# Features 128 to 191 of the output stacked by token halves before they are transposed, in a fused two-layer float32 kernel on one Trainium2 core

## The reference

```python
w = softmax(weight)                        # [8, 7], one row per 24 features
x = causal_conv7(x, w).reshape(8192, 192)
h = x @ w_in1;  x = (h / (1 + exp(-1.702 * h))) @ w_out1     # 192 -> 2048 -> 192
h = x @ w_in2
P = a[0] + a[1]*h + a[2]*h**2 + a[3]*h**3
Q = 1 + abs(b[0])*abs(h) + abs(b[1])*h**2
return (P / (Q + 1e-6)) @ w_out2           # [8192, 192]
```

## Time and profile before

| | |
|---|---|
| median of 3 runs | 1399.64 us (1399.02 to 1403.59) |
| profiled execution | 1398.76 us, span of its instructions 1396.6 us |
| granted TensorE clock, mean | 0.997 |
| PE, PEld, DVE, ACT, POOL busy | 1328.7, 706.6, 1107.6, 972.0, 326.5 us |

### The profile page before, as it was taken

The page is one execution under the profiler, slowest core; times in us unless marked ns, Lnnn a source line. Parts: engine busy times, 40 slices in busy tenths (PEclk is TensorE's granted clock), DMA queues, the critical chain, the costliest instruction groups (busy, mean ns, idle before and its releaser), DMA issues. The chain is left out here.

```text
span 1396.6 us, 14941 instructions
## 1 busy us (share of the span) xinstructions
PE 1328.7 (95%) x4896; PEld 706.6 (51%) x4896; DVE 1107.6 (79%) x1205; ACT 972.0 (70%) x1113; POOL 326.5 (23%) x150
## 2 busy tenths in 40 slices
PE   2999999999999999999999999999999999999886
PEld 1455555554555555555554555555455555555332
DVE  5229788887888888888888888888888888877885
ACT  4337777677777777677777767777677777766774
POOL 4202222222222222222222222222222222222222
PEclk9999999999999999999999999999999999999998
DMA  8100000000000000000000000000000000000000
GB/s 209 36 12 0 12 1 23 1 23 1 12 11 0 23 0 20 3 11 11 0 23 0 12 10 3 20 0 23 0 12 12 0 12 1 12 0 12 0 12 11
DMA packets 32884, 20.37 MB, mean 15 GB/s; under 512 B 10322, under 2 KB 30802, under 8 KB 32850
## 3 DMA queue, kind: packets, MB, share of 16 engines
q1 hardware_dynamic: 32372, 19.93, 5.2%
q10 hardware_dynamic: 477, 0.01, 0.0%
HBM read 13.64 MB, written 6.29 MB: 14 GB/s over the span
## 5 line engine op out<-in xcount | busy, mean ns | idle before, releaser
L675 POOL TENSOR_TENSOR work<-work 128x1024 f32<-128x1024 f32 x128 | 303.7, 2373 | 1013.2 <-ACT work L432 1010.1
L271 PE MATMUL acc_a<-g,down 128*128 128x512 f32 x1024 | 477.4, 607 | 0.0
L271 PEld LDWEIGHTS acc_a<-g,down 128*128 128x128 f32 x1024 | 183.4, 190 | 292.5 <-issue 292.5
L570 DVE TENSOR_TENSOR work<-work,h 128x1024 f32<-128x1024 f32 x128 | 156.3, 1221 | 195.8 <-ACT work L432 195.7
L277 PE MATMUL acc_b<-g,down 128*64 128x512 f32 x1024 | 270.9, 606 | 30.0 <-DVE x_a_lo L588 16.0
L428 ACT ACTIVATE work<-h,par 128x1024 f32<-128x1024 f32 x128 | 142.6, 1114 | 195.8 <-PE h L265 195.8
L257 PE MATMUL h<-x_a_hi,up_a_hi 128*128 128x512 f32 x512 | 234.6, 458 | 25.4 <-DVE x_b L560 16.8
L456 ACT ACTIVATE work<-work 128x1024 f32<-128x1024 f32 x128 | 135.9, 1061 | 156.1 <-POOL work L675 154.1
L258 PE MATMUL h<-x_a_lo,up_a_hi 128*128 128x512 f32 x512 | 201.2, 393 | 0.0
L259 PE MATMUL h<-x_a_hi,up_a_lo 128*128 128x512 f32 x512 | 200.6, 392 | 0.0
L260 PE MATMUL h<-x_b,up_b_hi 128*128 128x512 f32 x512 | 200.4, 392 | 0.0
(11 more groups left out here) (74 smaller groups left out, 967.4 us busy)
## 6 DMA issues: line engine op xcount, KB each, us to landing
out<-y_out SPq DMA_DIRECT2D x16, 384.0 KB, 2.5
x_in_a<-in_x SPq DMA_DIRECT2D x16, 256.0 KB, 2.8
down<-in_moe_w_out SPq DMA_DIRECT2D x8, 384.0 KB, 6.3
x_in_b<-in_x SPq DMA_DIRECT2D x32, 64.0 KB, 2.6
work<-in_moe_w_in SPq DMA_DIRECT2D x8, 256.0 KB, 6.0
work<-in_moe_w_in SPq DMA_DIRECT2D x16, 128.0 KB, 6.3
wts<-in_weight ACTq DMA_DIRECT2D x2, 0.4 KB
wts<-in_weight SPq DMA_DIRECT2D x2, 1.3 KB
```

The costliest lines, as they stand in the source:

```text
L271: last = mm(l.acc_a[:], l.down[:, f, 0:P], l.g[:, slot, k, :], start=f == 0, stop=f == STEPS - 1)
L570: tt(tu, tu, h, ALU.mult).then_inc(t2_ready, 1)
L675: tt(m, sq[(s - LAG_RATIO) % 2], seed, ALU.mult).then_inc(m_ready, 1)
```

## The change

`y_b` becomes 128 rows by 256 columns: rows 0 to 63 hold features 128 to 191 of tokens 0 to 255 of the tile, rows 64 to 127 the same features of tokens 256 to 511. Two copies of 64x256 on ACT fill it, and acc2_read counts to three a tile. Half h of a tile is then blocks 2h and 2h+1 for y_a, and columns 128h to 128h+127 of y_b, which hold blocks h and h+2: `transpose_y` has three transpositions of 128 columns and no product. ACT empties `turned` with two copies, 128x256 for the a part of blocks 2h and 2h+1, and 128x128 for the b part of blocks h and h+2, and y_ready counts to four a tile. The memset and its semaphore go.

```diff
-        y_b = sb("y_b", [P, NT])
+        y_b = sb("y_b", [P, HALF])
...
-                    wait(sp, y_ready, 2 * (i - 1))
+                    wait(sp, y_ready, 4 * (i - 1))
...
             def transpose_y(tile, half):
 
-                if isinstance(tile, int) and tile == 0:
-                    pe.wait_ge(y_b_cleared, 1)
-                wait(pe, acc2_read, 2 * (tile + 1))
+                wait(pe, acc2_read, 3 * (tile + 1))
                 for j in range(2):
-                    toks = slice((2 * half + j) * P, (2 * half + j + 1) * P)
-                    nc.tensor.transpose(turned[:, j * D:j * D + P], y_a[:, toks], ident[:])
-                    last = mm(turned[:, j * D + P:(j + 1) * D], y_b[:, toks], ident[:, 0:DB], start=True, stop=True)
-                last.then_inc(y_transposed, 1)
+                    block = 2 * half + j
+                    nc.tensor.transpose(turned[:, j * P:(j + 1) * P], y_a[:, block * P:(block + 1) * P], ident[:])
+                nc.tensor.transpose(turned[:, 2 * P:3 * P], y_b[:, half * P:(half + 1) * P], ident[:])\
+                    .then_inc(y_transposed, 1)
...
-                        wait(pe, y_ready, 2 * (tile - 3))
+                        wait(pe, y_ready, 4 * (tile - 3))
...
-                    wait(pe, y_ready, 2 * (i - 2) + half)
+                    wait(pe, y_ready, 4 * (i - 2) + 2 * half)
...
-                        wait(pe, acc2_read, 2 * (i - 1))
+                        wait(pe, acc2_read, 3 * (i - 1))
...
-                    fn(y_out[:, 2 * half:2 * half + 2, :],
-                       turned[:, 0:2 * D].rearrange("p (j d) -> p j d", d=D), ACT.Copy).then_inc(y_ready, 1)
+                    fn(y_out[:, 2 * half:2 * half + 2, 0:P],
+                       turned[:, 0:2 * P].rearrange("p (j d) -> p j d", d=P), ACT.Copy).then_inc(y_ready, 1)
+                    fn(y_out[:, half::2, P:D],
+                       turned[:, 2 * P:3 * P].rearrange("p (j d) -> p j d", d=DB), ACT.Copy).then_inc(y_ready, 1)
...
-                    fn(y_b[0:DB, :], acc_b[0:DB, :], ACT.Copy).then_inc(acc2_read, 1)
+                    fn(y_b[0:DB, :], acc_b[0:DB, 0:HALF], ACT.Copy).then_inc(acc2_read, 1)
+                    fn(y_b[DB:P, :], acc_b[0:DB, HALF:NT], ACT.Copy).then_inc(acc2_read, 1)
                     fn(y_a[:], L2.acc_a[:], ACT.Copy).then_inc(acc2_read, 1)
...
-            nc.vector.memset(y_b[DB:P, :], 0.0).then_inc(y_b_cleared, 1)
```

More of the change, by code:

```diff
@@ L163, in build_program @@
         s2_ready = sem("s2_ready"); z1_ready = sem("z1_ready"); z2_ready = sem("z2_ready")
-        g2_ready = sem("g2_ready"); g2_used = sem("g2_used"); y_b_cleared = sem("y_b_cleared")
+        g2_ready = sem("g2_ready"); g2_used = sem("g2_used")
         acc2_read = sem("acc2_read"); y_transposed = sem("y_transposed"); y_ready = sem("y_ready")
```

## The result

The changed kernel takes 1392.92 us (median of 6 runs, 1391.17 to 1396.26) against 1400.25 us before (6 runs): a ratio of 0.9948, 95% interval 0.9933 to 0.9963, or 7.3 us less. The forecast was 9.0 us less, 1390.6 us. The change makes the kernel faster, by the mechanism that was named, and by four fifths of the size.

A forecast was written before the change was run, and what follows sets the result against it. PE's own list bounds the kernel until about 1290 us. 28 halves x 0.33 gain 9.2 us, the tail loses 0.2; 1398.76 minus 9.0 is 1389.8, plus 0.9 to the median: 1390.6 us, range 1387.8 to 1394.4.

The forecast's parts named there:

- What bounds the kernel: Up to about 1290 us the time is the length of PE's own list; whatever leaves the list leaves the time.
- the rival of the hidden gain: A chain of ACT, POOL and DVE sets the period, so the gain is hidden: 1399.8 us, chance 0.02.
- Step 1: PE, y's transposition: two products (0.43 us) become one transposition (0.105); 0.33 us a half, 28 halves, 9.2 us gained.
- The rival that its price would be a product's: On PE, y_b's transposition costs what a float32 product costs: 6.2 us gained, 1393.6 us, chance 0.05.
- Step 2: ACT, y_b in two copies of 64x256: 0.40 us each, 0.80 instead of 0.48, 0.32 us more.
- Step 3: PE's first L277 of the next step waits for y_a: slack 0.30 us against 0.32 added, 0.02 x 14, nothing.
- Step 4: ACT, y_out in two copies per half: 0.1 us more overlapped, 0.4 without overlap; hidden from PE.
- Step 5: DVE loses one memset at the very start, needed only some 190 us later: nothing.
- Step 6: The end, ACT on the path: tile 14's copies +0.32, tile 15 together -0.14; tail +0.2 us.

The follow-up runs named there:

- the run with the split wait: Changed kernel, down projection's wait split: y_b's copies before the first L277, y_a only before layer 2's first L271; 1393.67 us, ratio 0.9948; repeated: 1391.01 us.
- the padded run: Kernel before, each product of y_b replaced by a transposition of all 128 rows (64 to 127 zeros), y_b not stacked; 1392.16 us, ratio 0.9953.
- the run with ACT's part alone: Kernel before, PE's list unchanged, y_b in two copies of 64x256 on partitions 0 to 63, y_out in two per half; 1398.9 us, ratio 0.9998.
- second profile: Changed kernel run once more, unedited; 1392.21 us, ratio 0.9956, span 1389.7 us.
- The stacked product: Changed kernel with the third transposition replaced by a float32 product of the stacked y_b with the whole identity; 1394.28 us, ratio 0.996.

## Why the prediction was right, and where its sizes were off

- **What bounds the kernel: right.** PE's list did. Every profiled span moved by what the run changed in the periods, within 0.9 us, and the rival of the hidden gain falls: steps of 10.47 went to 10.17 and stayed there.
- **Step 1, 0.33 us a half: measured 0.30** (28 halves give 8.4 us in the run with the split wait, where nothing else disturbs them; 9.2 were forecast). The price of the removed products (0.43 us) holds, since the padded run's 0.64 to 0.41 follows from it. The third transposition was forecast at 0.105 us and takes 0.12 to 0.13: 28 x 0.03 = 0.8 us less than forecast, the largest single miss of the sum. The rival that its price would be a product's fails; a product there costs 0.22.
- **Step 2, 0.32 us more on ACT for y_b: measured 0.31.** The reading that neighbours don't overlap where the starting partition changes was drawn from L441 and L411, and the run with ACT's part alone shows the contrast (0.26 against 0.39). The Trainium skill's bubble (Advanced Engine Details and Errata, The Read-Write Bubble) is visible here only at such a change. The Trainium skill (ScalarE: Activation LUTs, Rules for kernel authors) budgets about 0.3 us per ACTIVATE and 0.83 ns per element; for 256 columns that is 0.51 us, an estimate, against 0.36 to 0.38 measured; the 0.54 us that the two pages together gave is too much.
- **Step 3, the slack of 0.30 us: the size that failed relatively most.** Forecast 0.02 us x 14 = nothing; measured, the step is 0.03 to 0.04 us longer in ten tiles and 0.13 to 0.15 in four, 0.8 to 0.9 us together, of which some 0.4 us is left after the following steps. y_a's own copy became 0.02 us longer (0.60 after a copy to other partitions); that makes the usual tile's loss. The slack was read from one tile, and the four are other tiles: 0, 11, 12 and 13, whose copies stand outside the hardware loop. There L277 followed y_a's end by only 0.30 us in the kernel before, not by the 0.35 of tile 7, the one that was read:

```profile
1090.44 0.58 ACT L469 ACTIVATE y_a<-acc_a 128x512 f32<-128x512 f32 x1
1091.32 1.94 PE L277 MATMUL acc_b<-g,down 128*64 128x512 f32 x8
```

In the changed kernel L277 follows y_a's end by 0.10 us in these four (1089.67 to 1089.77) and by 0.05 in the others: 0.05 less slack and 0.05 more release. Why the release is longer there is open. A slack as large as the added time has no room for either.
- **Step 4: right.** y_out's pair costs 0.27 us to the second copy's start and 0.16 on from there, 0.06 us more in all, and PE's half 1 follows without a wait.
- **Step 5: right.** The start differs between the two profiles of the changed kernel by 4.5 us, and by nothing that the memset does.
- **Step 6, +0.2 us in the tail: +0.8 measured** (second profile: 7.7 us ahead at 1268.97, 6.9 at the end of the span). Up to the last full step, with tile 14's copies, 0.4 goes, where 0.32 was forecast. The very end was to give 0.14 back and gives nothing: ACT waits 1.4 us for the last transpositions instead of 1.8, 0.47 us gained where 0.66 were forecast, and y_b's and y_out's copies take that. The other 0.4 us no step of the prediction had, and it may be chance: in the first profile it is 0.1, in the padded run -0.3. After an idle time of 4.52 us PE comes back at half pace, and with the same instructions the upper pace returns at another place. PE's timeline in the kernel before:

```profile
1379.25 3.67 PE L277 MATMUL acc_b<-g,down 128*64 128x512 f32 x4 [4.52 <-DVE g L585]
1382.86 2.79 PE L271 MATMUL acc_a<-g,down 128*128 128x512 f32 x4
```

and in the second profile of the changed kernel:

```profile
1371.92 3.67 PE L277 MATMUL acc_b<-g,down 128*64 128x512 f32 x4 [4.52 <-DVE g L586]
1375.53 3.17 PE L271 MATMUL acc_a<-g,down 128*128 128x512 f32 x4
```

- Together, in the second profile: the steps with y -8.75 us, the steps before them +0.76, the other full steps +0.2, the tail +0.8, and the start +0.1 make the -6.9 us of the spans; the medians give -7.3, for -9.0 forecast. Of the 2.1 us that the spans lack, step 1 missed 0.8, step 3 some 0.4, step 6 0.6, and the rest is spread over other steps and the start. The medians' surplus of 0.4 us over the spans is within what the mixture of early and late starts moves.

What the prediction did not ask is which half of the idea works. The padded run has the mode without the stacking: it gains 6.3 us before the tail, costs ACT nothing, and ends at a span of 1389.8 us against the changed kernel's 1389.7. The stacked product has the stacking without the mode: 5.0 us before the tail. Both together give 7.8 there, counted from the first L271. Stacking on top of the mode is worth 0.07 us a half, 2.1 us, of which 0.4 go at L277 and 0.2 in other full steps. Nearly all the rest goes in the tail, which is 1.3 us longer than the padded run's: 0.3 at tile 14's copies, 0.3 at the very end, and 0.7 by where PE's upper pace returns, which may be chance. So these runs don't tell the padded and the stacked version apart.

## What to carry to other kernels

Price a small PE operation by the period of the step that has it against one that hasn't (the period runs from the first L271 of a step to that of the next), and look for the same operation elsewhere in the kernel: x's transpositions gave y's price within 0.02 us. When two engines meet at a wait that never shows, the slack is worth knowing to 0.05 us over many tiles, in the loop and outside it, and splitting a wait for several buffers into one per buffer cost nothing here. Before saving rows or columns of a tiny matmul, check that its neighbours have the same shape: carrying zeros along was cheaper by 15 us in the periods than changing between 128 and 64 rows.

## What the runs showed of the hardware that was not expected

- A change between operations on 128 and on 64 rows of the array costs 0.13 to 0.15 us (0.41, 0.66, 0.95 us for none, two, four changes around four transpositions).
- A float32 product of 128 rows costs 0.22 us with 128 moving columns and 0.215 with 64; a transposition of 128 columns 0.09 to 0.13, by how many stand in a row.
- On ACT the neighbour of a copy of 64x256 out of PSUM starts 0.26 us after it if both keep their partitions, 0.39 to 0.40 if one of them writes to partitions 64 to 127.
- After its idle time at the start PE ran at half pace until about 30 us in all profiles but one, and until about 41 us in that one, with the same instructions; this alone moved the execution by 4.5 us. Which of the two comes is open.
